# Setup of an attention and two-mixture kernel: outer rows set on chip, loads and constants in another order, narrower products of ones

## The chip, the cores and the metric

One Trainium2 chip, one of its cores. The metric is device time in microseconds (us) of one execution of the whole program.

## What is computed

Three parts follow one another; everything is float32. The change touches only what stands before the first one's loop.

```python
for t in range(S):                       # B=4, H=8, S=768, D=48
    kt, vt, rt = (k[:, :, t], v[:, :, t], r[:, :, t])
    cur = einsum('bhd,bhe->bhde', u * kt, vt)
    y[:, :, t] = einsum('bhd,bhde->bhe', rt, state + cur)
    state = w * state + einsum('bhd,bhe->bhde', kt, vt)
```

y becomes x (3072 tokens x 384). The first mixture forms softmax(x @ phi) over tokens and over slots, runs 32 slots through eight experts (384 to 1024 to 384) and mixes them back. The second sends each token to the expert of its largest x @ w_gate, scaled by that probability.

## The kernel before, in words

The recurrence is done in chunks of 128 tokens. Two heads with 48 features each sit on 96 of the 128 partitions (rows LO=16 to R2=112; the 16 rows on either side are unused), so there are 4 pairs of heads and 6 chunks, 24 steps (`pe_step`, L973), a loop of six chunks with four steps written out. In a step TensorE (PE) does `increments` (L932), `scores` (L920), the carried part (L943), `turn` (L963), `logits` (L968, with phi) and `within` (L954). Scores and within put their products on the four quadrants of the array in turn. Before a step VectorE (DVE) multiplies the loaded rows `ind` with a table of powers of w (`pre`, L637, giving `rkb`), and GpSimd (POOL) multiplies the token rows `intk` with the table's transpose `kttab` (L434, giving `kt`); ScalarE (ACT) multiplies by u (L486). `increments` waits for `kt` (L925), and POOL waits for `kttab`, `rkb` and the token rows (L429 to L432).

Setup has to bring this about, on five queues written out by hand; each engine runs its own in order.

- SyncE (SP), L309 to L323: w and u into `wusb` (96 rows, then the same small rows twice into the outer 16), the rows `ind` for steps 0 and 1 (`load_d`; step 0's misses the outer rows), four loads of phi, the gate's weights, token rows (`load_t`) and more `ind`.
- ACT, L462 to L467: waits for w and u, loads the outer rows of step 0's `ind` (`load_gaps`), loads its activation table, waits for the transposes and copies them to `kttab`.
- POOL, L412 to L423: the nine constants counted by `consts` (ones, ident, xs, two selects, fold, revi, sta, kt's margin), then `kt` of step 0.
- DVE, L606 to L650: memset of phi's unused rows, wait for all nine constants, masks, wait for w and u, six doublings of the table (L624 to L626, each on the last), `wk` (L642, L643), scaling of the table, `pre(0)`, `pre(1)`.
- PE, L888 to L901: 15 products of ones (`warm`, 128x128 each, their result unused), five products of xs that clear PSUM banks, the four transposes of `wk`, eight more products of ones, a wait for phi and the gate's weights, step 0.

Of the kernel before, what the change touches and what calls it, by code (L numbers as in the profile page):

```python
# [12 lines left out]
P = 128  # L13
# [6 lines left out]
R2 = HB + D  # L20
LO = HB - D
# [5 lines left out]
NS = E * SPE  # L27
# [8 lines left out]
def mixed_kernel(nc, dmaj, tmaj, wu, phi, wa, wg, wb, out):  # L36
    ctx = ExitStack()
    with ctx:
# [13 lines left out]
        def sem(name):  # L52
            return ctx.enter_context(nc.semaphore(name))
# [13 lines left out]
        xs = sb("xs", [P, B, C])  # L67
# [37 lines left out]
        ones = sb("ones", [P, P])  # L105
# [64 lines left out]

        zeroed = sem("zeroed")
        consts = sem("consts")
        wu_in = sem("wu_in")
        small_in = sem("small_in")
# [107 lines left out]
        PARTS = ((0, 3), (3, 6))  # L282
        NCONST = 9
# [7 lines left out]
        def _(sp):  # L291
            drows = dmaj.rearrange("n r i c -> (n r) i c")

            def load_d(n):

                row = (n // PAIRS + n % PAIRS * NC) * 2 * D  # L300
                if row >= LO and row + P - LO <= STEPS * 2 * D:
                    sp.dma_start(ind[:, n % 4, :, :], drows[row - LO:row - LO + P, 0:2]).then_inc(ind_in[n % 4], 16)
                else:
                    sp.dma_start(ind[LO:R2, n % 4, :, :], drows[row:row + 2 * D, 0:2]).then_inc(ind_in[n % 4], 16)

            def load_t(n):
                sp.dma_start(intk[:, n % 4, :, :, :], step_of(tmaj, n)).then_inc(tok_in[n % 4], 16)

            sp.dma_start(wusb[LO:R2, :, :], wu[:]).then_inc(wu_in, 16)  # L309
            sp.dma_start(wusb[0:LO, :, :], wu[0:LO]).then_inc(wu_in, 16)  # L310
            sp.dma_start(wusb[R2:P, :, :], wu[0:LO]).then_inc(wu_in, 16)
            load_d(0)
            load_d(1)
# [4 lines left out]
            sp.dma_start(wgsb[:, :, :], wg).then_inc(small_in, 16)  # L318
            load_t(0)
# [84 lines left out]
        def _(pool):  # L404
# [3 lines left out]
            def step(ins):  # L408
                n[0] += 1
                ins.then_inc(consts, 1)  # L410
# [3 lines left out]
            step(g.memset(xs[:, :, :], 0.0))  # L414
# [4 lines left out]
                                 base=0, pattern=[[-1, P]], channel_multiplier=1))  # L419
            step(g.memset(fold[:, :], 0.0))  # L420
# [28 lines left out]
        def _(sc):  # L449
# [12 lines left out]
            sc.wait_ge(wu_in, 48)  # L462
# [132 lines left out]
        def _(dve):  # L595
# [5 lines left out]
            def link(ins):  # L601
                chain[0] += 1
                ins.then_inc(dch, 1)
                dve.wait_ge(dch, chain[0])

            v.memset(phisb[32:64, :, :, :], 0.0).then_inc(zeroed, 1)  # L606
            v.memset(tab[:, :, 1, HALF - 1:HALF], 1.0)
            dve.wait_ge(consts, NCONST)
# [9 lines left out]
            dve.wait_ge(wu_in, 48)  # L618
# [10 lines left out]
            def scale_tables(a, b):  # L629
                inv = winv[0:P, a:b].unsqueeze(2).unsqueeze(3).to_broadcast([P, b - a, 2, HALF])  # L630
                return v.tensor_tensor(tab[0:P, a:b, :, :], tab[0:P, a:b, :, :], inv, ALU.mult)
# [13 lines left out]
            link(scale_tables(0, 1))  # L645
            pre(0)
# [231 lines left out]
        def _(pe):  # L878
# [4 lines left out]
            def warm(n, bank):  # L883

                for _ in range(n):
                    mm(ps[:, bank, 0:P], ones[:, :], ones[:, :], start=True, stop=True)  # L886

            pe.wait_ge(consts, 1)  # L888
            warm(15, SC)
            pe.wait_ge(consts, NCONST)  # L890

            for bank in (YB, YB + 1, SB, SB + 1, LB):
                mm(ps[:, bank, 0:B * HALF], xs[0:R2, 0, :], xs[0:R2, 0:2, :].rearrange("p b t -> p (b t)"),
                   start=True, stop=True)
            pe.wait_ge(wk_ready, 1)
# [4 lines left out]
            warm(8, SC)  # L900
            pe.wait_ge(small_in, 5 * 16)  # L901
# [210 lines left out]
            turn_c(4)  # L1112
            for k in range(KD):
                pe.wait_ge(sot_ready, k + 1)
                ins = mm(ps[:, 3, 0:E], sot[:, k, :], wgsb[:, k, :], start=(k == 0), stop=(k == KD - 1))
# [140 lines left out]
```

## Time and profile before

| | |
|---|---|
| median of three runs | 281.63 us (279.12 to 281.95) |
| profiled execution, its own time | 280.6 us |
| span of the profiled execution | 278.8 us |
| mean granted clock of TensorE | 0.978 of full speed |
| PE busy | 260.8 us, 94% of the span |
| DVE busy | 153.2 us, 55% |
| chain that ended last | PE 81%, DVE 13%, issue 3% |
| HBM read and written | 50.32 MB and 4.72 MB |

The span goes from the first to the last instruction. The granted clock is a share of 2.4 GHz. "issue" in a chain is time in which an engine waited for nothing that the profile shows. A product of ones or of xs is recorded as two instructions.

### The profile page before, as it was taken

To read this page: it belongs to the slowest core of one execution; us is meant where nothing else is said; L and a number is where in the kernel's file an instruction comes from. 1 tells how busy PE (TensorE), PEld (TensorE's weight loads), DVE (VectorE), ACT (ScalarE), POOL (GpSimd) and SP (SyncE) were. 2 spreads that over 40 slices of the span, in tenths; PEclk is the share of its full clock that TensorE was granted. 3 is DMA by queue.
4 is the path that set the end of the run, shared out by engine and by line. 5 is a ranking of instruction groups with operands and counts; after the bars stand their busy time and mean duration, and the time that the engine had idled before them with its cause. 6 is when DMAs were issued, how large, how long until landed. Compare 5 with 4: busy or idle time off the path is not lost.

```text
span 278.8 us, 10399 instructions
## 1 busy us (share of the span) xinstructions
PE 260.8 (94%) x4505; PEld 220.9 (79%) x4505; DVE 153.2 (55%) x296; ACT 88.7 (32%) x175; POOL 30.5 (11%) x45
## 2 busy tenths in 40 slices
PE   8989799989999998999999989999999999999992
PEld 8967687877788775433468679999999999999991
DVE  5787488888888876247021487342522524425203
ACT  1224254544555544030220273222222222222200
POOL 3222122222222124000000000000000000000000
PEclk9999799999999999999997799999999999999998
DMA  5975889999999999999804700030030300300303
GB/s 158 331 241 171 256 321 322 394 363 395 385 360 365 319 405 418 423 385 414 364 2 155 298 2 1 0 114 0 0 113 0 113 0 0 113 0 1 114 0 119
DMA packets 16324, 55.30 MB, mean 198 GB/s; under 512 B 1936, under 2 KB 5200, under 8 KB 15408
## 3 DMA queue, kind: packets, MB, share of 16 engines
q1 hardware_dynamic: 13216, 43.90, 42.6%
q10 hardware_dynamic: 3088, 11.14, 10.7%
q8 instruction: 12, 0.20, 0.3%
q14 instruction: 8, 0.07, 0.1%
HBM read 50.32 MB, written 4.72 MB: 197 GB/s over the span
## 4 chain that ended last, share of the span: by engine, by line
PE 81%; DVE 13%; issue 3%; ACT 1%; POOL 0%; DVEq 0%; POOLq 0%
PE ps L1183 12%; PE ps L1182 12%; PE ps L1184 12%; PE ps L920 9%; PE ps L954 6%; DVE pt L669 6%; PE ps L886 5%; DVE pt L666 5%; PE ps L932 4%; PE ps L1167 4%; PE ps L1054 4%; PE ps L1076 4%; PE ps L1023 2%; PE ps L1085 1%; PE ps L1124 1%
## 5 line engine op out<-in xcount | busy, mean ns | idle before, releaser
L1183 PE MATMUL ps<-w2l,hh 128*128 128x384 f32 x192 | 64.5, 336 | 0.0
L1182 PE MATMUL ps<-w2h,hh 128*128 128x384 f32 x192 | 64.4, 335 | 0.0
L821 DVE SCALAR_TENSOR_TENSOR hl<-ps,hh 128x512 fp32r<-128x512 f32 x48 | 32.9, 689 | 57.1 <-ACT hh L567 57.1
L1184 PE MATMUL ps<-w2h,hl 128*128 128x384 f32 x192 | 64.2, 335 | 0.0
L567 ACT ACTIVATE hh<-ps 128x512 fp32r<-128x512 f32 x48 | 28.7, 600 | 74.1 <-PE ps L1167 74.1
L1183 PEld LDWEIGHTS ps<-w2l,hh 128*128 128x128 f32 x192 | 36.0, 188 | 1.6
L1182 PEld LDWEIGHTS ps<-w2h,hh 128*128 128x128 f32 x192 | 36.0, 188 | 0.7
L1184 PEld LDWEIGHTS ps<-w2h,hl 128*128 128x128 f32 x192 | 36.1, 188 | 0.0
L434 POOL TENSOR_TENSOR kt<-intk,kttab 128x384 f32<-128x384 f32 x24 | 24.1, 1006 | 74.7 <-DVE rkb L637 50.0
L637 DVE TENSOR_TENSOR rkb<-ind,tab 128x1024 f32<-128x1024 f32 x24 | 29.9, 1246 | 1.4 <-DMA ind<-dmaj 1.3
L920 PE MATMUL ps<-rkb 64*64 64x128 f32 x768 | 27.5, 279 | 0.0
L666 DVE TENSOR_TENSOR pt<-ps,mask 128x512 f32<-128x512 f32 x24 | 16.6, 692 | 12.5 <-PE ps L920 12.5
L500 ACT ACTIVATE xs<-ps 112x512 f32<-112x512 f32 x24 | 14.3, 597 | 26.5 <-PE ps L954 26.5
L920 PEld LDWEIGHTS ps<-rkb 64*64 64x64 f32 x768 | 22.2, 135 | 0.0
L954 PEld LDWEIGHTS ps<-pt,intk 64*48 64x48 f32 x768 | 13.2, 119 | 11.3 <-issue 11.3
L943 PE MATMUL ps<-rkb,stb 64*48 64x64 f32 x384 | 21.0, 224 | 0.0
L954 PE MATMUL ps<-pt,intk 64*48 64x64 f32 x768 | 16.4, 220 | 4.7 <-DVE pt L669 3.6
L943 PE MATMUL ps<-rkb,sta 64*48 64x64 f32 x384 | 20.6, 224 | 0.0
L1167 PE MATMUL ps<-cs,gst 128*128 (+1 forms) x48 | 18.7, 395 | 1.6 <-DVE gst L809 1.1
L943 PEld LDWEIGHTS ps<-rkb,sta 64*48 64x48 f32 x384 | 15.6, 122 | 3.5 <-issue 0.3
L886 PE MATMUL ps<-ones 128*128 128x128 f32 x80 | 16.9, 372 | 1.3 <-POOL ident L413 1.3
L669 DVE COPY_PREDICATED pt<-diag,ps 128x512 f32<-128x512 int32 x24 | 17.6, 733 | 0.8
(163 smaller groups left out, 308.1 us busy)
## 6 DMA issues: line engine op xcount, KB each, us to landing
ind<-dmaj SPq DMA_DIRECT2D x22, 512.0 KB, 8.0
wearly<-wa ACTq DMA_DIRECT2D x21, 512.0 KB, 7.4
intk<-tmaj SPq DMA_DIRECT2D x24, 384.0 KB, 7.1
wearly<-wa SPq DMA_DIRECT2D x4, 1536.0 KB, 10.0
out<-acc SPq DMA_DIRECT2D x5, 768.0 KB, 3.6
wlate<-wa SPq DMA_DIRECT2D x4, 768.0 KB, 8.3
wlate<-wa SPq DMA_DIRECT2D x2, 1536.0 KB, 10.7
wmid<-wa SPq DMA_DIRECT2D x1, 1536.0 KB, 8.0
```

Of the source, the lines that this page charges most:

```text
L637: v.tensor_tensor(rkb[0:P, n % 4, 0:2, :].rearrange("p i (g t) -> p i g t", t=HALF), ind[0:P, n % 4, :, :].rearrange("p i (g t) -> p i g t ...
L666: v.tensor_tensor(pt[:, :, :, :], score[:, :, :, 0, :], causal, ALU.mult).then_inc(pt_ready, 1)
L669: v.copy_predicated(pt[:, :, :, :], on_diag, score[:, :, :, 1, :]).then_inc(att_ready, 1)
L821: v.scalar_tensor_tensor(out=hl[:, f % 4, :], in0=ps[:, f % 4, :], scalar=0.0, in1=hh[:, f % 4, :].bitcast(F32), op0=ALU.max, op1=ALU.subt ...
L886: mm(ps[:, bank, 0:P], ones[:, :], ones[:, :], start=True, stop=True)
L920: ins = mm(ps[toks[m], SC + j, b * C:(b + 1) * C], rkb[toks[j], ip, 1, at_], rkb[toks[j], ip, 0::2, at_], start=True, stop=True, skip_grou ...
L943: ins = mm(ps[rows[j ^ b % 2], YB + m, b * HALF:(b + 1) * HALF], st[toks[j], ip, b, :], rkb[toks[j], ip, 0, b * C + m * HALF:b * C + (m + ...
L954: ins = mm(ps[rows[j ^ b % 2], YB + m, b * HALF:(b + 1) * HALF], intk[toks[m], ip, 1, b, j * D:(j + 1) * D], pt[toks[m], j, b, :], start=F ...
L1167: mm(ps[:, f % 4, :], gst[:, f * P:(f + 1) * P], cs[:, bass.ds(u * (UT * P), UT * P)], start=True, stop=True).then_inc(h_done, 1)
L1182: mm(o, a_h, w2h[:, f, :], start=(f == 0), stop=False)
L1183: mm(o, a_h, w2l[:, f, :], start=False, stop=False)
L1184: ins = mm(o, a_l, w2h[:, f, :], start=False, stop=(f == KF - 1))
```

## The change

DVE sets the outer rows of `wusb` to 1.0 itself, in two memsets (rows 0 to 31 and 96 to 127), ahead of everything else, and signals it by `sides_set`; the two loads of these rows go. SP issues step 0's `ind` first, then waits for `sides_set`, then loads the 96 rows of w and u, then step 0's token rows; step 1's `ind` goes behind phi. The gate's weights get a semaphore of their own, for which PE waits only where it needs them. ACT no longer waits for w and u in front of the outer rows of `ind`. POOL sets xs behind the two selects, and DVE's masks wait for four constants instead of nine; the wait for nine stands in front of `pre(0)`. The products of ones shrink to 32x32, and 79 in three places stand where 23 stood in two.

```diff
+            load_d(0)
+            sp.wait_ge(sides_set, 1)
             sp.dma_start(wusb[LO:R2, :, :], wu[:]).then_inc(wu_in, 16)
-            sp.dma_start(wusb[0:LO, :, :], wu[0:LO]).then_inc(wu_in, 16)
-            sp.dma_start(wusb[R2:P, :, :], wu[0:LO]).then_inc(wu_in, 16)
-            load_d(0)
-            load_d(1)
+            load_t(0)
             sp.wait_ge(zeroed, 1)
...
-            sp.dma_start(wgsb[:, :, :], wg).then_inc(small_in, 16)
-            load_t(0)
+            load_d(1)
+            sp.dma_start(wgsb[:, :, :], wg).then_inc(wg_in, 16)
...
-            step(g.memset(xs[:, :, :], 0.0))
             pool.wait_ge(consts, n[0])
...
+            step(g.memset(xs[:, :, :], 0.0))
...
-            sc.wait_ge(wu_in, 48)
             load_gaps()
...
+            v.memset(wusb[0:32, :, :], 1.0)
+            v.memset(wusb[96:P, :, :], 1.0).then_inc(sides_set, 1)
             v.memset(phisb[32:64, :, :, :], 0.0).then_inc(zeroed, 1)
             v.memset(tab[:, :, 1, HALF - 1:HALF], 1.0)
-            dve.wait_ge(consts, NCONST)
+            dve.wait_ge(consts, NSHAPE)
...
-            dve.wait_ge(wu_in, 48)
+            dve.wait_ge(wu_in, 16)
...
             link(scale_tables(0, 1))
+            dve.wait_ge(consts, NCONST)
             pre(0)
...
-            def warm(n, bank):
+            def warm(n, bank, width=P):
 
                 for _ in range(n):
-                    mm(ps[:, bank, 0:P], ones[:, :], ones[:, :], start=True, stop=True)
+                    mm(ps[0:width, bank, 0:width], ones[:, 0:width], ones[:, 0:width], start=True, stop=True)
 
             pe.wait_ge(consts, 1)
-            warm(15, SC)
+            warm(24, SC, NS)
...
+            warm(28, SC, NS)
             pe.wait_ge(wk_ready, 1)
...
-            warm(8, SC)
-            pe.wait_ge(small_in, 5 * 16)
+            warm(27, SC, NS)
+            pe.wait_ge(small_in, 4 * 16)
...
             turn_c(4)
+            pe.wait_ge(wg_in, 16)
```

NSHAPE is 4, NS 32, P 128.

PE's instructions from the start up to step 0, first as they stood and then as they stand now. A row is a line of the kernel, the operation, what it writes and from what, its shape, and how many in a row; `ps<-ones` are the products of ones, `ps<-xs` those that clear banks, `ps<-ident,wk` the transposes.

```order
0 L877 UNCONDITIONAL_BRANCH
1 L886 MATMUL ps<-ones 128x128 x15
2 L893 MATMUL ps<-xs 128x256 x5
3 L897 MATMUL ps<-ident,wk 128x112 x4
4 L886 MATMUL ps<-ones 128x128 x8
5 L990 UNCONDITIONAL_BRANCH
```

```order
0 L881 UNCONDITIONAL_BRANCH
1 L890 MATMUL ps<-ones 32x32 x24
2 L897 MATMUL ps<-xs 128x256 x5
3 L890 MATMUL ps<-ones 32x32 x28
4 L902 MATMUL ps<-ident,wk 128x112 x4
5 L890 MATMUL ps<-ones 32x32 x27
6 L995 UNCONDITIONAL_BRANCH
```

A third group has come between the clearing products and the transposes, and all three are narrow.

SyncE's issues at the start, as they stood and as they stand now: `wusb<-wu` is w and u, `ind<-dmaj` the rows for DVE (96 or 128 partitions), `phisb<-phi` phi, `wgsb<-wg` the gate's weights, `intk<-tmaj` token rows.

```order
2 L309 DMA wusb<-wu 96x8
3 L310 DMA wusb<-wu 16x8
4 L311 DMA wusb<-wu 16x8
5 L304 DMA ind<-dmaj 96x1024
6 L302 DMA ind<-dmaj 128x1024
7 L316 DMA phisb<-phi 48x128 [waits zeroed]
8 L317 DMA phisb<-phi 48x128
9 L316 DMA phisb<-phi 48x128
10 L317 DMA phisb<-phi 48x128
11 L318 DMA wgsb<-wg 128x24
12 L307 DMA intk<-tmaj 128x768 x2
```

```order
2 L307 DMA ind<-dmaj 96x1024
3 L314 DMA wusb<-wu 96x8 [waits sides_set]
4 L310 DMA intk<-tmaj 128x768
5 L318 DMA phisb<-phi 48x128 [waits zeroed]
6 L319 DMA phisb<-phi 48x128
7 L318 DMA phisb<-phi 48x128
8 L319 DMA phisb<-phi 48x128
9 L305 DMA ind<-dmaj 128x1024
10 L321 DMA wgsb<-wg 128x24
11 L310 DMA intk<-tmaj 128x768
```

Step 0's rows have moved ahead of w and u, its token rows ahead of phi, and step 1's rows behind phi.

## Rows read from the trace of the kernel before

**Rows 1.** Chain of waits, first 40 us: start, us, what ran or was waited for.
```profile
1.27 6.36 PE ps L886 x30
7.63 2.16 PE ps L893 x10
9.79 0.38 PE ps L897 x4
10.17 1.80 PE ps L886 x16
...
12.09 0.62 PE ps L932 x23
...
19.82 0.75 issue
...
27.97 1.35 issue
```

**Rows 2.** Timeline, 0 to 24 us: start, us, engine, line, operation, out<-in, count, idle before.
```profile
3.21 0.87 ACTq L455 DMA_DIRECT2D ind<-dmaj  x2
3.21 0.17 DVE L613 TENSOR_TENSOR tab<-strict 128x4 f32<-128x4 f32 x1 [1.45 <-POOL kt L423]
...
4.04 0.16 DVE L619 TENSOR_TENSOR uw<-wusb 128x4 f32<-128x4 f32 x1
...
7.20 0.42 DVE L643 TENSOR_TENSOR wk<-tab,pw 128x256 f32<-128x256 f32 x1
...
7.47 2.32 PE L893 MATMUL ps<-xs 112*128 112x256 f32 x10
...
9.26 1.23 DVE L637 TENSOR_TENSOR rkb<-ind,tab 128x1024 f32<-128x1024 f32 x1 [1.32 <-DMA ind<-dmaj]
...
10.21 0.49 ACT L467 ACTIVATE kttab<-ps 128x384 f32<-128x384 f32 x1 [4.60 <-PE ps L897]
...
10.84 1.00 POOL L434 TENSOR_TENSOR kt<-intk,kttab 128x384 f32<-128x384 f32 x1 [7.66 <-ACT kttab L467]
...
15.31 0.66 PE L954 MATMUL ps<-pt,intk 64*48 64x64 f32 x32
...
15.77 0.76 PE L932 MATMUL ps<-intk,kt 64*64 64x48 f32 x32
```

**Rows 3.** Timeline of later steps, the same columns, 19 to 40 us.
```profile
24.01 0.99 PE L954 MATMUL ps<-pt,intk 64*48 64x64 f32 x32 [0.17 <-DVE pt L669]
...
30.38 0.62 PE L932 MATMUL ps<-intk,kt 64*64 64x48 f32 x30 [0.17 <-issue]
...
35.40 0.63 PE L932 MATMUL ps<-intk,kt 64*64 64x48 f32 x32
...
39.06 0.66 PE L932 MATMUL ps<-intk,kt 64*64 64x48 f32 x32
```

**Rows 4.** DMA view, 0 to 40 us: a queue's packets; issues by size, us to landing.
```profile
q8 instruction: 4, 0.07, 0.6%
...
ind<-dmaj SPq DMA_DIRECT2D x10, 512.0 KB, 5.7
...
ind<-dmaj SPq DMA_DIRECT2D x1, 384.0 KB, 4.2
...
phisb<-phi SPq DMA_DIRECT2D x4, 24.0 KB, 4.7
...
wusb<-wu SPq DMA_DIRECT2D x1, 3.0 KB, 1.6
```

**Rows 5.** Windows (PE, PEld, DVE, ACT, POOL busy, PEclk, DMA); line L1124.
```profile
31.00:32.00 1.00, 1.00 (x28) 1.00 (x24) 0.41 (x1) 0.49 (x1) 0.00 (x0) 0.50 0.94 156
147.00:150.40 3.40, 3.06 (x28) 3.06 (x28) 0.73 (x5) 0.29 (x1) 0.00 (x0) 1.00 0.07 18
150.50:153.00 2.50, 2.50 (x14) 2.50 (x13) 0.00 (x0) 0.00 (x0) 0.00 (x0) 0.50 0.90 344
...
L1124 PE MATMUL ps<-gw,cs x24: 252/253/354, 147.3 to 152.9; 128*128 128x8 f32 x24
```

More of the change, by code:

```diff
@@ L168, in mixed_kernel @@
         ltok = flat[:, 0:NC * P].rearrange("p (c b s) -> p c b s", c=NC, b=B)
+        sides_set = sem("sides_set")
         zeroed = sem("zeroed")
@@ L173, in mixed_kernel @@
         wu_in = sem("wu_in")
+        wg_in = sem("wg_in")
         small_in = sem("small_in")
@@ L282, in mixed_kernel @@
         PARTS = ((0, 3), (3, 6))
+        NSHAPE = 4
         NCONST = 9
```

## The prediction

> **What bounds the kernel now.** I read the chain of waits first, over the first 40 us [rows 1]: it is almost wholly TensorE (PE). PE runs products of ones from 1.27, five products of xs from 7.63, four transposes of the table from 9.79, eight more products of ones from 10.17, and begins step 0 at 12.09. The 15 products of ones are 30 records of an instruction, two per product, and last 6.36 us; the later eight, 16 records, last 1.80. One record costs 0.212 us in the first run and 0.112 in the second: PE began on its lower level, 1.2 GHz, and went over to 2.4 GHz. Solving 30 records over the 6.20 us from 1.27 to the first xs record at 7.47 [rows 2] for the two prices (28 slow, 2 fast) puts the change at 7.2 us; the granted clock, which reads 1.00 from the start, does not show it.
>
> The timeline of setup [rows 2] shows who else is near. VectorE (DVE) starts its table at 3.21, when GpSimd's (POOL) ninth constant is there, reaches the powers at 4.04, ends wk at 7.62, and then sits idle for 1.32 us until the first rows of ind land at 9.26; that product ends at 10.49. ScalarE copies the table from 10.21 to 10.70, POOL multiplies it into kt from 10.84 to 11.84, PE starts step 0 at 12.09. So two arms nearly tie for kt: PE's (transposes end 10.17, 1.92 us before step 0) and DVE's (product ends 10.49, 1.60 before). A shortened wait counts only if both move.
>
> After setup nothing in the change touches a step. A step undisturbed takes 3.66 us (35.40 to 39.06), and steps wait on PE and DVE by turns, not on setup [rows 3]. So what setup gains is carried to the end once. Span 278.8 plus 1.8 us around it make this execution's 280.6.
>
> **DVE's arm, part by part.** The wait for nine constants becomes a wait for four, and xs's memset goes behind the two selects, so the table's first product leaves 3.21 for about 2 us. Its masks are 0.83 us of work (3.21 to 4.04) and end before 3.2 even if that start were 2.4. What ends last is then w and u, whatever these edits bring. Before, their three loads went out first, landed 1.6 us after issue (the last at about 3.3) and cost nothing. Now the one load waits for two short memsets on DVE (issue about 1.55), and on SyncE's queue it stands behind 384 KB of ind issued at the program's start, 0.8. The queue gives small loads no way past: phisb's 24 KB loads, issued behind 896 KB of ind, took 4.7 us where wusb took 1.6 [rows 4]. The same 384 KB took 4.2 us. So w and u land at 0.8 + 4.2 = 5.0, plus an estimated 0.2 for the gap rows that ScalarE now issues at the same moment: 5.2. Were they held by nothing, 1.55 + 1.6 = 3.15; behind a load as slow as the whole ind rows (5.7), 6.5. I take 5.2, as its row is the same transfer.
>
> DVE so reaches the powers 1.16 us later than before (5.2 against 4.04). wk ends at 8.78, the table's first part is scaled by 9.1 (7.62 to 7.94 before, where the idle time begins). The wait for ind goes, as its three loads, issued at 0.8 to 1.2 instead of up to 3.65, are there by 6.9 even at 5.7 us each. The first product runs 9.12 to 10.35, and POOL can start 0.14 later (as 10.70 to 10.84): 10.49. Step 0 is 1.25 behind POOL's start: 11.74. What replaces the idle 1.32 is w and u: the DVE arm gains 0.2 to 0.35 and no more. The two ends of the landing would put step 0 at 9.7 and at 13.0.
>
> **PE's arm.** 15 products of 128 columns go, 24 of 32x32 come. No row shows such a product. Eight records follow one another in each quadrant of L954 (32 records on four): start to start of the next group 0.46 us, 0.0575 each for 64 columns, against half of 0.112 = 0.056 [rows 2]. So the price goes by columns, plus about 0.002: for 32 columns 0.030 a record, 0.06 a product at 2.4 GHz and 0.11 at 1.2. The other end is that narrowness saves nothing: L1124's moving side has 8 columns, yet the window it shares with 128-wide ones holds 28 records in 3.06 us, 0.109 each [rows 5]. Those have 128 columns to load, the new ones 32, so I stay by L954.
> - 24 x 0.11 = 2.64: PE reaches the xs products at 3.91 (the ninth constant comes at 3.2 as before, since POOL's total is unchanged).
> - They now run on the lower level, where they cost twice 2.16/5 = 0.43. Until 7.2 that is 3.29/0.86 = 3.8 products, then 1.2 x 0.43 = 0.50: end at 7.70 instead of 9.79.
> - 28 x 0.06 = 1.68: 9.38. wk is ready at 8.78, so these products are 0.6 too many here.
> - Transposes 0.38: 9.76, 0.41 us before the old 10.17. Copy, kt and step 0 follow 1.92 later: 11.68.
> - The last run is 27 x 0.06 = 1.62 instead of 1.80: it ends at 11.38, inside the wait for kt.
>
> The two arms give 11.74 and 11.68 against 12.09: **0.35 to 0.41 us gained**, 0.4 taken. If the small price is exact in columns (0.056), PE's arm is at 11.5 and DVE's decides; if the clock rises later, both kernels lose half of the delay.
>
> The Trainium skill, "TensorE: Matmul & The Clock Gate", section "The mechanism" of the part on packing small matmuls, says that a weight load overlaps running products only when the row group differs. All products of ones use the same rows. The trace disagrees: in 3.40 us of products of ones and of the gate, loads and products are each busy for 3.06 [rows 5]. By the rule, small loads and products would take turns; that is rival 2 below.
>
> **Other edits.** The moved load of ind for step 1 is issued at about 4.3 instead of 2.63, behind token rows and phi. Whole ind loads took 5.7 us, so it lands by 10.0; DVE wants it at 10.35 + 0.55 = 10.9. Cover is 0.9 us; gone, step 1 would wait that much. Token rows of step 0 are issued at about 2.0, ahead of phi: even at 5.7 they are there by 7.7, wanted at 10.5. SyncE issues two small loads fewer and waits once more, all off the path. phi is issued from 2.5 to 4.2, earlier than before by half a microsecond, and at 4.7 lands by 9, wanted at 11.4. The gate's own semaphore is passed 130 us after its load: 0. Rows of w set to one change no work. Unseen and not bounded by the order alone: 56 more products move the places at which PE's instruction queue is refilled. Three stalls that end for no releaser (0.75 at 19.82, some 0.3 in L954 at 24.01, where the group lasts 0.99 against 0.66, and 1.35 at 27.97) come while instruction packets are on the rings: four in 40 us [rows 3, 4]. After the last, the granted clock fell to 0.50 by 31 [rows 5], and step 4 lasted 5.02 (30.38 to 35.40), 1.36 over a free step. These bound what a shift could do: -0.75 - 1.35 - 1.36 = -3.5 to, with one stall and one slow step more, +2.7. I take 0, since a step has 72 products and the stalls stand a little under a step apart (19.82, within 24.01 to 25.00, 27.97), so 56 more in front moves each place by nearly one spacing, onto its neighbour's.
>
> The Trainium skill, "Runtime: NRT & Kernel Launch", section "Instruction fetch mechanics", says that an engine's instructions are refilled in blocks by transfers of their own, and that crossing a block's edge is mostly hidden. By that rule the shift costs nothing and the stalls are of another cause. No row settles it; 1.35 us is not hidden if it is a refill.
>
> **Rivals.**
> 1. The forecast: both arms by 0.4. 280.6 - 0.4 = 280.2; on the mean of the four executions shown (three times and the profiled one, 280.8) it is 280.4.
> 2. Small products take load and stream in turn: 0.12 a product, 0.22 slow. 24 x 0.22 to 6.55; xs to 9.0; 28 x 0.12 to 12.4; transposes to 12.8; 27 x 0.12 to 16.0, step 0 there instead of at 12.09: +3.9, 284.7. For it: no row shows narrow products one after another on the same rows. Against: L954. At no saving at all, 24 products end at 9.5, xs at 11.6, the rest at 24.2: +12, the end of that bound.
> 3. Slower by the clock: the small runs and the 0.3 us hole behind them fail to hold 2.4 GHz, the granted clock falls around step 0 and one step lasts 1.36 more. 280.8 - 0.4 + 1.36 = 281.8. It decides if PE is off 2.4 GHz at 12 us. For it: in 147 to 150.4 PE was busy for 3.06 of 3.40 us, every second product or so with 8 columns moving, and the clock was at 0.50 from 150.5 all the same [rows 5]. Against: the first run of ones raised it, and load and product are equally wide in both kinds.
> 4. Refills fall elsewhere: all three losses gone, 280.4 - 3.5 = 276.9; or one stall and slow step more, 283.1.
> 5. w and u are not held by ind: DVE's arm is at 9.7, but PE's stays at 11.68, so again 280.4. That the change does less than meant on DVE hides behind PE, and the other way round.
>
> **How the numbers follow.** Forecast (with rival 5) 0.53; rival 2 0.06; rival 3 0.18; rival 4 faster 0.15, slower 0.08. Time 280.4. The likeliest's own range is 279.2 to 281.6, the scatter of its arms and of the executions. The range leaves out rival 2 and the outer edge of rival 4: 277.6 to 283.0. A measurement of this kernel can tell about 1% from no change: faster by over 1% is rival 4's good side and a little of the forecast's scatter, 0.18; slower by over 1%, rival 2 and part of rival 4, 0.11; within, 0.71.
>
> **What would show it.** Right: DVE's uw starts at 5.0 to 5.5 with ind's load of 96 rows just landed; no idle before the first rkb; xs products from 3.9 with long records; about 0.06 us a small product after 7.2; step 0's L932 group at 11.6 to 11.8; then steps of 3.66. Wrong: uw before 4.5 and step 0 before 11.3; transposes later than 10.2; a granted clock of 0.50 before 20 us; stalls without a releaser that sum to 1 us more or less than 2.4.

## The result, and the profile after

The change made the kernel slower: 283.62 us median of 20 executions (281.68 to 287.15) against 281.29 of 20 before (277.12 to 282.35). The ratio is 1.0119, 95% interval 1.0092 to 1.0146. A ratio is made of the undisturbed executions alone, a median of all, so the two can point apart. The profiled execution took 283.61, its span 281.9, its mean granted clock 0.979: 3.0 above the one of before, so it stands for the medians' 2.3 with 0.7 of scatter.

Lines have moved: products of ones are L890 (before L886), xs L897, transposes L902, increments L937 (L932), scores L925, the carried part L948, logits L973, within L959 (L954), `kt` L436, `rkb` L640. The timeline of the changed kernel's setup, columns as in [rows 2]:

```profile
1.27 2.74 PE L890 MATMUL ps<-ones 128*32 128x32 f32 x48 [1.27 <-POOL ident L415]
...
3.94 4.00 PE L897 MATMUL ps<-xs 112*128 112x256 f32 x10
...
5.22 0.16 DVE L622 TENSOR_TENSOR uw<-wusb 128x4 f32<-128x4 f32 x1 [2.03 <-DMA wusb<-wu]
...
7.87 1.96 PE L890 MATMUL ps<-ones 128*32 128x32 f32 x56
...
9.16 1.22 DVE L640 TENSOR_TENSOR rkb<-ind,tab 128x1024 f32<-128x1024 f32 x1
9.75 0.60 PE L902 MATMUL ps<-ident,wk 112*128 112x112 f32 x4
...
10.89 1.23 DVE L640 TENSOR_TENSOR rkb<-ind,tab 128x1024 f32<-128x1024 f32 x1
11.02 2.90 POOL L436 TENSOR_TENSOR kt<-intk,kttab 128x384 f32<-128x384 f32 x2 [7.76 <-ACT kttab L468]
```

Up to here it is nearly the forecast's setup. The wait of DVE for the first rows of `ind` is gone, and a wait of 2.03 us for w and u stands in its place. What the forecast does not have is the last row's length: two `kt` products one behind the other, 2.90 us. The line's own view gives their durations, shortest, median and longest in ns, and who waited:

```profile
L436 POOL TENSOR_TENSOR kt<-intk,kttab x2: 994/1468/1943, 11.0 to 12.9; 128x384 f32<-128x384 f32 x2
...
  PE ps L937: 1.0, 1
```

The chain of waits of the changed kernel, 0 to 45 us (columns as in [rows 1]), says where the rest is:

```profile
9.82 0.55 PE ps L902 x4
...
11.02 1.95 POOL kt L436
...
13.22 0.62 PE ps L937 x23
...
17.43 0.45 PE ps L937 x23
17.88 2.17 issue
20.05 0.20 PE ps L937
...
28.02 0.66 PE ps L959 x31
28.68 0.53 issue
29.21 0.25 PE ps L959
...
32.66 0.44 PE ps L959 x14
33.11 0.62 issue
```

Step 0 starts at 13.22 instead of 12.09. Then PE stops three times for nothing that the profile shows, once for 2.17 us behind the 31st of the 32 records of `increments` of step 1; before it was 0.75, 0.3 and 1.35 at other places [rows 1, 3]. The windows of those microseconds, columns as in [rows 5]:

```profile
17.00:18.00 1.00, 0.88 (x62) 0.75 (x53) 1.00 (x1) 0.49 (x1) 0.00 (x0) 1.00 1.09 385
18.00:19.00 1.00, 0.00 (x0) 0.00 (x0) 0.05 (x1) 0.81 (x2) 0.87 (x1) 1.00 0.78 311
...
20.00:21.00 1.00, 0.91 (x24) 0.74 (x27) 0.41 (x1) 0.00 (x0) 0.00 (x0) 0.90 0.02 8
21.00:22.00 1.00, 1.00 (x32) 1.00 (x26) 0.11 (x1) 0.00 (x0) 0.00 (x0) 0.50 0.08 16
```

The stall begins while `ind` and token rows fill the DMA engines (385 and 311 GB/s), and behind it the granted clock falls to 0.50. So step 1 lasts from 17.22 to 24.79, 7.57 us: a free step of 3.66, the stall of 2.17 and 1.74 more. Step 5, where the rows of `increments` show both kernels running freely again (after, then before at 35.40 in [rows 3]):

```profile
38.18 0.66 PE L937 MATMUL ps<-intk,kt 64*64 64x48 f32 x32
```

That is 2.78 us later than before: 1.13 of it stood at step 0, 1.65 came in steps 0 to 4. The 1.65 is a difference of two rounds that both have stalls: the stalls sum to 3.3 against 2.4, the step with the clock at 0.50 costs 1.74 against 1.36, and step 0 lasts 4.00 against 3.68. Nearly the whole 3.0 of the two profiled executions is therefore there by 38 us.

### The profile page after: what moved, and what is told of

Read it like the earlier page. It is cut to its first block, busy times and chain, and to the rows that moved or that the text cites. A ratio compares the mean times of both kernels' runs of the same rounds, so it can differ in the third digit from the quotient of the medians.

```text
span 281.9 us, 10624 instructions
## 1 busy us (share of the span) xinstructions
PE 260.9 (93%) x4617; PEld 219.4 (78%) x4617; DVE 153.6 (54%) x298; ACT 88.8 (32%) x175; POOL 31.4 (11%) x45
## 4 chain that ended last, share of the span: by engine, by line
PE 76%; DVE 14%; issue 4%; DMA 2%; ACT 1%; POOL 1%; SPq 1%; DVEq 0%; POOLq 0%
PE ps L1189 12%; PE ps L1188 12%; PE ps L1190 12%; PE ps L925 9%; DVE pt L673 6%; PE ps L959 6%; DVE pt L670 6%; PE ps L937 4%; PE ps L1173 4%; PE ps L1059 4%; PE ps L1081 4%; DMA wraw<-wb 2%; PE ps L890 2%; PE ps L1028 2%; PE ps L897 1%
## 5 line engine op out<-in xcount | busy, mean ns | idle before, releaser
L1189 PE MATMUL ps<-w2l,hh 128*128 128x384 f32 x192 | 65.2, 340 | 0.0
L1188 PE MATMUL ps<-w2h,hh 128*128 128x384 f32 x192 | 65.1, 339 | 0.0
L1189 PEld LDWEIGHTS ps<-w2l,hh 128*128 128x128 f32 x192 | 36.6, 191 | 1.7
L1188 PEld LDWEIGHTS ps<-w2h,hh 128*128 128x128 f32 x192 | 36.6, 191 | 0.7
L436 POOL TENSOR_TENSOR kt<-intk,kttab 128x384 f32<-128x384 f32 x24 | 25.0, 1043 | 76.4 <-DVE rkb L640 53.2
L640 DVE TENSOR_TENSOR rkb<-ind,tab 128x1024 f32<-128x1024 f32 x24 | 29.2, 1219 | 0.1
L925 PE MATMUL ps<-rkb 64*64 64x128 f32 x768 | 27.7, 277 | 0.1
L925 PEld LDWEIGHTS ps<-rkb 64*64 64x64 f32 x768 | 22.1, 134 | 2.8 <-issue 2.8
L959 PEld LDWEIGHTS ps<-pt,intk 64*48 64x48 f32 x768 | 13.3, 119 | 11.4 <-issue 11.4
L959 PE MATMUL ps<-pt,intk 64*48 64x64 f32 x768 | 16.5, 220 | 5.2 <-DVE pt L673 4.1
L948 PE MATMUL ps<-rkb,stb 64*48 64x64 f32 x384 | 21.1, 225 | 0.0
L948 PE MATMUL ps<-rkb,sta 64*48 64x64 f32 x384 | 20.8, 225 | 0.0
L1173 PE MATMUL ps<-cs,gst 128*128 (+1 forms) x48 | 19.6, 416 | 1.1 <-DVE gst L813 0.7
L937 PE MATMUL ps<-intk,kt 64*64 64x48 f32 (+1 forms) x768 | 16.0, 212 | 4.4 <-issue 3.3
L948 PEld LDWEIGHTS ps<-rkb,sta 64*48 64x48 f32 x384 | 15.7, 122 | 3.5 <-issue 0.3
```

What stands on the lines that cost most here:

```text
L640: v.tensor_tensor(rkb[0:P, n % 4, 0:2, :].rearrange("p i (g t) -> p i g t", t=HALF), ind[0:P, n % 4, :, :].rearrange("p i (g t) -> p i g t ...
L925: ins = mm(ps[toks[m], SC + j, b * C:(b + 1) * C], rkb[toks[j], ip, 1, at_], rkb[toks[j], ip, 0::2, at_], start=True, stop=True, skip_grou ...
L948: ins = mm(ps[rows[j ^ b % 2], YB + m, b * HALF:(b + 1) * HALF], st[toks[j], ip, b, :], rkb[toks[j], ip, 0, b * C + m * HALF:b * C + (m + ...
L959: ins = mm(ps[rows[j ^ b % 2], YB + m, b * HALF:(b + 1) * HALF], intk[toks[m], ip, 1, b, j * D:(j + 1) * D], pt[toks[m], j, b, :], start=F ...
L1173: mm(ps[:, f % 4, :], gst[:, f * P:(f + 1) * P], cs[:, bass.ds(u * (UT * P), UT * P)], start=True, stop=True).then_inc(h_done, 1)
L1188: mm(o, a_h, w2h[:, f, :], start=(f == 0), stop=False)
```

## The experiments

Two things are to be told apart: the hold of `kt` on POOL, and the stalls without a releaser. My theory of the stalls was that they are refills of PE's instruction queue, at fixed counts of products; its rival, that they come from the moment, by what the loads and the other engines do then. "In front" below is the number of products of any kind before step 0: 32 before the change (15 + 5 + 4 + 8) and 88 after (24 + 5 + 28 + 4 + 27). A step has 72: 16 of `increments`, 16 of `scores`, 8 carried, 4 of `turn`, 8 carried, 4 of `logits`, 16 of `within`, each recorded twice but for the four of `turn`. Each ratio is to the kernel before, run beside the kernel in question.

**e1_hold**: DVE's second product is kept behind POOL's first.

```diff
+            dve.wait_ge(kt_ready, 1)
             pre(1)
```

> The changed kernel, with DVE made to wait for kt of step 0 before its second ind product. Theory A (the first kt product took 1.94 us instead of 1.00 because DVE's second ind product, started 0.13 us ahead of it, kept it from working): the first kt product lasts 1.00 again and step 0 starts at about 12.25 instead of 13.22; the second ind product ends at about 13.3 instead of 12.1. The time falls by about 1.0 us against the changed kernel. Rival R (that product was long for another reason, late token rows or its first use): it stays at 1.9 us, and step 0 starts at 13.2 or later. Either way the stall of about 2.2 us in increments of step 1 stays.

Measured: 283.09 us, ratio to before 1.0144 (1.0077 to 1.0211). Its timeline of setup:

```profile
10.42 0.49 ACT L468 ACTIVATE kttab<-ps 128x384 f32<-128x384 f32 x1 [7.21 <-PE ps L903]
...
11.05 1.00 POOL L436 TENSOR_TENSOR kt<-intk,kttab 128x384 f32<-128x384 f32 x1 [7.79 <-ACT kttab L468]
12.14 1.23 DVE L640 TENSOR_TENSOR rkb<-ind,tab 128x1024 f32<-128x1024 f32 x1 [1.18 <-issue]
```

`kt` takes 1.00 again, and step 0 comes at 12.30, 0.92 earlier. Before the change the same pair met the other way round, and it was DVE's product that became long (timeline of the kernel before, behind POOL's start at 10.84 in [rows 2]):

```profile
10.98 1.93 DVE L637 TENSOR_TENSOR rkb<-ind,tab 128x1024 f32<-128x1024 f32 x1
```

So whichever of the two starts first is done in its own time (1.23 or 1.00), and the other ends 0.85 (POOL behind DVE) or 1.07 us (DVE behind POOL) after it. 0.13 us of order decides over 0.94 us of `kt`. Yet the kernel is no faster: its chain has stalls of 2.18 at 13.43 and 1.90 at 19.12.

**e2_refill** and **e3_both**: eight products more in the third run, without and with e1's wait.

```diff
-            warm(27, SC, NS)
+            warm(35, SC, NS)
```

> The changed kernel with 35 instead of 27 small products in the third run, so 64 instead of 56 more products than before in front of step 0. Theory B (PE's instructions are refilled every 64 products, and where the boundary falls in a step sets the stall): the stalls return to the places of the kernel before: about 0.75 at the end of within of step 1, some 0.3 in within of step 2, about 1.35 in logits of step 3, and the 2.17 in increments of step 1 is gone. Step 0 still starts near 13.2 (the third run ends about 12.8). Steps 1 to 4 last together about 1 to 1.5 us less than in the changed kernel. Rival R (stalls come from the DMA traffic of these moments, not from the place in the program): the 2.2 us stall stays in increments of step 1, and the time is the same or worse by the eight products.

> Both edits of e1 and e2 together. Theories A and B: step 0 at about 12.8 to 13.0 (the third run of ones now ends about 12.8 and decides), stalls at the old places; the time is about 1.5 to 2 us under the changed kernel and equal to the kernel before within 1 us. If neither theory holds: as the changed kernel.

Measured: 282.91, ratio 1.0133 (1.0071 to 1.0195), and 283.68, ratio 1.0116 (1.0044 to 1.0188). The stalls moved and the 2.17 is gone: e2 stands still for 1.68 in front of `scores` of step 0 (its chain counts 1.02 of it, at 13.65), 1.29 at 22.29 and 0.76 at 32.05. That sums to 3.7 against 3.3, so nothing was saved. With 96 in front the edges, the products at which a refill is due, lie at the old places within the steps, but each is a later piece of the program than before. A miss for "the places alone decide".

**e4_wu_first**: w and u issued ahead of step 0's `ind`.

```diff
-            load_d(0)
             sp.wait_ge(sides_set, 1)
             sp.dma_start(wusb[LO:R2, :, :], wu[:]).then_inc(wu_in, 16)
+            load_d(0)
```

> The changed kernel with w and u loaded ahead of step 0's ind instead of behind it. Theory C (w and u were held by the 384 KB in front of them, and the DVE arm follows their landing): uw starts at about 3.2 instead of 5.22, wk ends at 6.8, the first ind product at about 8.5. PE's arm stays (transposes at 9.75, kt product from 11.0), and as DVE's second ind product is over before or soon after 11.0, kt needs 1.0 to 1.4 us: step 0 at 12.3 to 12.7 instead of 13.22. Rival R (w and u land late for another reason, such as the wait for the memsets): uw stays near 5.

Measured: 283.49, ratio 1.0186 (1.0124 to 1.0248). The powers start at 3.53 instead of 5.22, so the 384 KB in front did hold this load; `wk` is there by 7.1, step 0 starts at 11.90. Then `increments` of step 1 stalls for 2.18 again, and nothing of the 1.3 us is left in the median.

**e5_pe_alone** and **e6_rest_alone** split the change: the kernel before with the new products of ones only, and the change without them (15 and 8 wide ones as before). **e12_rest_again** is e6 again, on another chip.

> The kernel before with only PE's products changed (24, 28 and 27 narrow ones in three places). Theory B, now as e1 to e3 left it (an instruction refill is asked for when PE passes an edge, every 64 products, and is there 4 to 6 us later; 79 quick products in setup use one up early, so the first round of the loop is paced by refills whatever the other arms do): step 0 starts at about 12, stalls stand in scores of step 0 or increments of step 1 as in the changed kernel, step 5 starts near 38 instead of 35.4, and the time is 2 to 3 us over before, nearly all of the change's loss. Rival A (the loss is DVE's second ind product holding up kt, which needs the DVE side of the change): here kt comes first as before, so the time is that of before.

> The change without PE's part: 15 and 8 products of 128 columns as before, all the rest changed. Theory B: stalls where the kernel before has them (end of within of step 1, within of step 2, logits of step 3), step 5 within 0.7 us of 35.4, time within 1 us of before; uw at about 5.2. Step 0 at 12.1 if kt starts ahead of DVE's second ind product, at 13.1 if behind it, and then 0 to 1 us longer in all. Rival: the moved loads cost the time; then this kernel is as slow as the changed one, and step 0 or a later step waits on DMA.

> The same kernel as e6 (the change without PE's part), for a profile without a disturbed clock and to bound its gain, as it measured 1.1% under before. Expected: 0.5 to 1.3% under before again. If the gain is from setup, step 0 starts before 12.0; if it is from the stalls, steps 1 to 4 together last under 22 us against 23.3 before.

Measured: e5 283.47, ratio 1.0108 (1.0045 to 1.0171); e6 279.43, ratio 0.9891 (0.9843 to 0.9939); e12 280.64, ratio 1.0019 (0.9915 to 1.0122). The new products of ones, by themselves, lose as much as the whole change. The rest gives nothing that holds up: e6's 1% did not come back. The chain of e5, in which setup's loads are those of before:

```profile
12.61 0.51 PE ps L921 x15
13.12 0.59 issue
...
16.77 0.45 PE ps L933 x23
17.22 2.18 issue
19.40 0.20 PE ps L933
...
28.05 0.97 issue
```

The same product of step 1 stalls for the same 2.18, at another time (17.22) and behind other loads. That is the sign of a count, not of a moment.

**e7_few_wide**: seven long products instead of the 79, which keep PE busy with less of its program (16 in front; `width` columns read from one column of ones).

```diff
-                    mm(ps[0:width, bank, 0:width], ones[:, 0:width], ones[:, 0:width], start=True, stop=True)
+                    mm(ps[:, bank, 0:width], ones[:, :], ones[:, 0:1].to_broadcast([P, width]), start=True, stop=True)
...
-            warm(24, SC, NS)
+            warm(3, SC, 256)
...
-            warm(28, SC, NS)
+            warm(2, SC, 512)
...
-            warm(27, SC, NS)
+            warm(2, SC, 512)
```

> The changed kernel with its 79 narrow products replaced by 7 wide ones of about the same length (3 of 256 columns, then 2 and 2 of 512), so 16 products stand in front of step 0 instead of 88. Theory B: the first edge falls at the end of scores of step 0 and only three refills stand in the loop's first round instead of five; stalls of about 1 us each near step 1's scores, step 2's and step 3's, step 5 at 35 to 36, time 2 to 3.5 us under the changed kernel, at or under before. Rival A: step 0 is again held by kt (13.1) and the time stays that of the changed kernel.

Measured: 286.41, ratio 1.0173 (1.0109 to 1.0237), the slowest of the timed kernels: "fewer products, fewer stalls" fell. Timeline of e7 (PE), and its windows:

```profile
16.60 0.66 PE L925 MATMUL ps<-rkb 64*64 64x128 f32 x14
19.04 0.70 PE L925 MATMUL ps<-rkb 64*64 64x128 f32 x17 [1.78 <-issue]
...
21.95 0.66 PE L937 MATMUL ps<-intk,kt 64*64 64x48 f32 x30
26.39 0.32 PE L937 MATMUL ps<-intk,kt 64*48 64x48 f32 x2 [3.78 <-issue]
```

```profile
23.00:24.00 1.00, 0.00 (x0) 0.00 (x0) 0.00 (x0) 0.53 (x1) 0.85 (x1) 1.00 0.80 320
24.00:25.00 1.00, 0.00 (x0) 0.00 (x0) 0.00 (x0) 0.00 (x0) 0.00 (x0) 1.00 0.00 0
25.00:26.00 1.00, 0.00 (x0) 0.00 (x0) 0.00 (x0) 0.00 (x0) 0.00 (x0) 0.71 0.00 0
26.00:27.00 1.00, 0.61 (x10) 0.56 (x13) 0.26 (x1) 0.00 (x0) 0.00 (x0) 0.50 0.00 0
```

From 24 to 26 every engine and every DMA engine is idle. One instruction packet (the DMA view's q8) starts between 23.80 and 23.95, when the loads are through, and PE goes on 2.4 to 2.6 us later. The clock falls within that idle time.

**e8_no_middle**: no second run (60 in front).

> The changed kernel without the 28 products of the middle run, so 60 in front of step 0. Transposes follow wk at about 8.9 instead of 9.75, kt starts near 10.5 ahead of DVE's second ind product, step 0 at about 11.8. Theory B: the first edge is passed in the third run (about 10.3), so step 0 stalls near its turn (about 15.3) and step 5 starts near 36, some 2 us less than the changed kernel. Rival A alone: no stall but those of before, 1.4 us less than the changed kernel. Rival C (the middle run is needed to hold the clock): the granted clock reads 0.50 somewhere from 9 to 16 us and step 0 is longer by over 1 us.

Measured: 282.87, ratio 1.0057 (1.0017 to 1.0098), step 0 at 12.95. Its windows show what the second run is good for:

```profile
8.00:9.00 1.00, 0.00 (x0) 0.00 (x0) 0.93 (x5) 0.00 (x0) 0.00 (x0) 1.00 1.25 356
9.00:10.00 1.00, 0.81 (x4) 0.60 (x4) 0.93 (x3) 0.00 (x0) 0.00 (x0) 0.65 0.74 284
10.00:11.00 1.00, 1.00 (x19) 0.94 (x19) 1.00 (x2) 0.74 (x2) 0.04 (x1) 0.50 0.99 368
```

PE is idle for 1.87 us before the transposes, from 7.32; the clock goes down in the slice from 9 to 10 and stays at 0.50 into 12 us.

**e9_mixed** (24 narrow, then 4 and 8 products of 128 columns; 45 in front) and **e10_mixed_wu_first** (the same with e4's order of loads):

```diff
-            warm(28, SC, NS)
+            warm(4, SC)
...
-            warm(27, SC, NS)
+            warm(8, SC)
```

> The changed kernel with its first run left at 24 narrow products, its middle run of 28 narrow ones made 4 of 128 columns and its third of 27 made 8 of 128 columns: the same lengths in time (0.89 and 1.8 us), but 45 products in front of step 0 instead of 88. Theory B (what costs is the number of products, since PE's instructions come in pieces of 64 products and each piece needs 2.3 us and its wait on the rings): edges fall at places 3 and 67 of step 0, then late in steps 1 to 3, four pieces in the first round instead of five; stalls sum to 2 to 2.7 us, none over 1.5; step 5 at 34.5 to 36; the time is 2 to 4 us under the changed kernel and equal to or under before. Rival R (narrow products cost by something else than their number, for instance the clock they hold): the first run is still narrow, so the time stays within 1 us of the changed kernel.

> e9 with w and u also loaded ahead of step 0's ind. DVE's arm: uw at 3.5, first ind product from about 7.5, second from about 9.5 when its rows land. PE's arm: transposes at about 8.2 to 9, kt from about 9.5, 1.0 us if it starts ahead of DVE's second ind product and up to 1.4 if behind. Step 0 at 10.6 to 11.5, about 1 us before e9's. Theory B with refills paced by the ring: part of that microsecond is given back in stalls; the time is 0 to 1 us under e9. If stalls did not follow, the full microsecond shows.

Measured: 280.3, ratio 1.0029 (0.9966 to 1.0092), and 280.76, ratio 1.0053 (0.9989 to 1.0116). Step 0 starts at 12.14 and 10.28: 1.86 us of a shorter setup bring nothing. Step 5 starts at 36.02 and 34.72.

**e11_long_run**: 91 narrow products in the third run, so that the count passes an edge where PE waits for no data. This is the most direct of the runs.

```diff
-            warm(27, SC, NS)
+            warm(91, SC, NS)
```

> The changed kernel with 91 instead of 27 narrow products in its third run, 64 more, to see a refill by itself. Theory B: the second edge lies after the 51st product of that run, where no step and no other engine plays a part; PE stops there for 1 to 2.5 us in the middle of like instructions, until some 2.3 us after an instruction packet starts on the rings. The next edge is at the 24th product of step 0 with one more stall of 1 to 2 us. Rival R (the stalls come from what the steps wait for): the run of 91 goes through in 6.4 us without a gap.

One execution, 287.86. Timeline of e11, and of its DMA view the window 11.9 to 12.0 (a queue's packets, MB, share of the engines):

```profile
9.95 3.48 PE L890 MATMUL ps<-ones 128*32 128x32 f32 x104
14.37 2.65 PE L890 MATMUL ps<-ones 128*32 128x32 f32 x78 [0.94 <-issue]
...
20.80 0.66 PE L937 MATMUL ps<-intk,kt 64*64 64x48 f32 x31
24.17 0.24 PE L937 MATMUL ps<-intk,kt 64*48 64x48 f32 x1 [2.72 <-issue]
```

```profile
q8 instruction: 1, 0.02, 58.4%
```

Between two like products with nothing between them PE stands still for 0.94 us, behind the 52nd of the run (104 records of two a product), which is the 113th of the program (24 + 5 + 28 + 4 + 52). The packet starts 2.4 us before PE goes on. The products there wait for no data and no other engine, and the granted clock reads 1.00 from 12 to 15. Counted the same way from records, give or take one where records are missing, every long stall lies 64 products, or a multiple of 64, from the others:

| kernel | in front | stall at | products up to it |
|---|---|---|---|
| after | 88 | 17.88 | 88 + 72 + 15.5 = 175.5 |
| after | 88 | 28.68 | 88 + 144 + 71.5 = 303.5 |
| after | 88 | 33.11 | 88 + 216 + 56 + 7 = 367 |
| e5 | 88 | 13.12 | 88 + 16 + 7.5 = 111.5 |
| e7 | 16 | 17.26, 22.61 | 16 + 72 + 16 + 7 = 111, 16 + 144 + 15 = 175 |
| e11 | 152 | 13.43, 21.45 | 113, 152 + 72 + 15.5 = 239.5 |

About 112, 176, 240, 304, 368: the same edges in every kernel, and the number in front says which product of a step they hit. The Trainium skill, "Runtime: NRT & Kernel Launch", section "Instruction fetch mechanics", gives a block as 16 KiB or 256 instructions. At two loads and two products for a float32 product that is the 64 seen here, and the packets have 0.02 MB: on the size the runs agree. The section also says that crossing an edge is mostly hidden; here it was not, with 0.94 us inside a run and 3.78 in a step.

**e13_old_places** (32 in front as before, made of 3 x 256, 2 x 512 and 1 x 512 columns and 17 narrow ones) and **e14_old_places_wu_first** (the same with e4's order):

```diff
-            warm(24, SC, NS)
+            long(3, SC, 256)
...
-            warm(28, SC, NS)
+            long(2, SC, 512)
...
-            warm(27, SC, NS)
+            long(1, SC, 512)
+            warm(17, SC, NS)
```

> The changed kernel with its runs of ones kept at about their lengths in time but made of 3 products of 256 columns, 2 of 512, and 1 of 512 with 17 narrow ones: 32 products in front of step 0, as before, instead of 88. Theory B' (the loss is where the refill edges fall in the steps: 64 products apart, and an edge at place 16 of a step after step 0 costs about 2 us or more, since it is asked for right behind the wait for DVE and while the next step's rows are on the rings): edges at 8, 72, 64 and 56 as before; no stall of over 1.6 us; time within 1% of before, 2 to 4 us under the changed kernel. Rival (the small and quick run itself costs, or the loads' new order): the time stays by the changed kernel's.

> e13 with w and u loaded ahead of step 0's ind. Step 0 at 10.3 to 10.8 against 12.1 in the kernel before. Theory B': edges as before, so 0.5 to 1.5 us under before, the rest given back where a refill comes later than the step. If it is the same as e13, all that setup gains is given back to the refills.

Measured: 281.08, ratio 1.0006 (0.9975 to 1.0037), and 279.18, ratio 0.9974 (0.9939 to 1.001). The chain of e14:

```profile
11.54 0.62 PE ps L943 x24
...
23.16 0.89 issue
...
27.51 0.53 issue
```

The old number in front gives the old time, with the new loads and the new order of constants. (e2 and e3 have the old places too, and not the old time.) The two stalls of e14 are 1.42 in all, step 5 starts at 32.79, and its median is the lowest of all, 1.8 below that of before as run beside it. By the ratio the gain is not proved: its interval includes 1.

**e15_before_moved**: the kernel before with 24 in front (11 of 128 and 2 of 256 columns, then 2 of 512 in place of 8), nothing else.

> The kernel before with nothing changed but how its ones are cut: 11 of 128 columns and 2 of 256 instead of 15 of 128, and 2 of 512 instead of 8 of 128; the same time, but 24 products in front of step 0 instead of 32, so every edge comes eight places later: 24 of step 0, 16 of step 1, 8 of step 2, 0 and 64 of step 3. Theory B': a stall of about 2 us or more in increments of step 1 as in the changed kernel, step 0 unchanged at 12.1, and 1 to 3 us over before. Rival (what costs is the number of products in front): fewer of them, so the same time as before or less.

Measured: 282.41 against 280.97 by the medians, but the ratio is 0.9964 (0.9922 to 1.0005). Half of the forecast failed. With 24 in front the edges lie at the same places of a step as with 88, yet nothing stands still at place 16 of step 1, where the changed kernel loses 2.17; a stall of 3.58 comes at 20.14, one edge later (24 + 144 + 7 = 175), in `increments` of step 2. So stalls keep to the edges, but the place in a step does not set the price of one, and by the ratio this kernel is not slower than before.

The timed kernels side by side. "Step 0" and "step 5" are the starts of their `increments`, "lost" is what five steps took over five free ones, 18.3, and "packets" are those of PE's queue in the whole execution; these four are read from the one profiled execution, whose time stands beside them and can lie well off the median (e2, e14):

| kernel | in front | packets | step 0 | step 5 | lost | profiled | median | ratio |
|---|---|---|---|---|---|---|---|---|
| before | 32 | 12 | 12.09 | 35.40 | 5.0 | 280.6 | 281.3 | 1 |
| e13 | 32 | 12 | 12.70 | 33.95 | 3.0 | 281.9 | 281.1 | 1.0006 |
| e14 | 32 | 12 | 11.54 | 32.79 | 3.0 | 276.4 | 279.2 | 0.9974 |
| e6 | 32 | 12 | 12.36 | 34.72 | 4.1 | 281.9 | 279.4 | 0.9891 |
| e12 | 32 | 12 | 12.10 | 34.35 | 4.0 | 279.2 | 280.6 | 1.0019 |
| e9 | 45 | 12 | 12.14 | 36.02 | 5.6 | 282.1 | 280.3 | 1.0029 |
| e10 | 45 | 12 | 10.28 | 34.72 | 6.1 | 281.7 | 280.8 | 1.0053 |
| e8 | 60 | 13 | 12.95 | 36.37 | 5.1 | 282.0 | 282.9 | 1.0057 |
| after | 88 | 13 | 13.22 | 38.18 | 6.7 | 283.6 | 283.6 | 1.0119 |
| e1 | 88 | 13 | 12.30 | 38.99 | 8.4 | 284.0 | 283.1 | 1.0144 |
| e4 | 88 | 13 | 11.90 | 36.91 | 6.7 | 283.0 | 283.5 | 1.0186 |
| e5 | 88 | 13 | 11.99 | 37.71 | 7.4 | 283.0 | 283.5 | 1.0108 |
| e2 | 96 | 13 | 12.31 | 37.56 | 7.0 | 286.5 | 282.9 | 1.0133 |
| e3 | 96 | 13 | 12.40 | 39.18 | 8.5 | 284.2 | 283.7 | 1.0116 |
| e15 | 24 | 12 | 12.26 | 37.55 | 7.0 | 284.3 | 282.4 | 0.9964 |
| e7 | 16 | 12 | 12.45 | 40.08 | 9.3 | 285.4 | 286.4 | 1.0173 |

Four kernels with 88 in front start step 0 at anything from 11.90 to 13.22 and have medians of 283.1 to 283.6. The number in front groups the ratios: within 0.6% of before from 24 to 60 (apart from e6's 0.9891, which did not come back), 1.1% to 1.9% over it at 88 and 96. The start of step 0 does not. e7, with 16, fits no such order. What comes behind the loop plays no part in this: it took 169.5 to 173.0 us in all sixteen, 171.1 before and 171.6 after.

The packets say more on why the number counts. PE's queue over the whole execution (packets, MB, share of the engines), first before, then after:

```profile
q8 instruction: 12, 0.20, 0.3%
```

```profile
q8 instruction: 13, 0.21, 0.3%
```

In the first 45 us, the first round of the loop and a little more, they start at 13.5, 18.1, 22.2 and 27.0 before, and at 11.9, 17.7, 21.9, 26.8 and 31.3 after; the next ones come at 65.0 and 67.3. The ones at about 18, 22 and 27 serve the same three edges in both, at nearly the same times, and PE gets past the edge near product 304 at 29.32 before and at 29.21 after. But after, 56 of these products were ones in place of work of the steps. At 3.66 us for the 72 products of a free step, 56 are 2.85 us (an estimate); step 5 came 2.78 later. My reading is that in this round the packets set the pace as well as the engines, and that a shorter setup (e1, e4) is given back there. No run shows it by itself, and the estimate is a rough one: it is right to 0.5 us for e8 and e9 and off by over a microsecond for e2, e4 and e10, the four other kernels with 32 in front reach step 5 by 0.7 to 2.6 before the kernel before does, and for e15 and e7 it has the wrong sign.

## Why the prediction was wrong

I forecast 280.4, no change; it was 283.6, slower by 1.2%. Two steps failed.

1. **"I take 0, since a step has 72 products and the stalls stand a little under a step apart"**: the term for the shifted refills. The observation was right and what I made of it wrong. The spacing is 64 products; 56 more in front is one spacing less 8, so the places are the neighbours' to within 8 products. But that like places cost alike is what failed: e2 and e3 have exactly the old places, one spacing on, and are 1.2% to 1.3% slower, and e15 has the places of the changed kernel and is not. What the shift did was to put 56 products of ones into the pieces that the first round is fed with. In the changed kernel that showed as 2.17 us at the end of `increments` of step 1 and, behind it, a clock of 0.50. The term measured +1.65 over steps 0 to 4 in the profiled execution, within the bound of +2.7 that I gave and then set aside. e5, which has the products of ones and not the hold of `kt`, is 1.1% slower by itself, and e13, which has the rest of the change and the old number, is not slower (1.0006).
2. **"POOL can start 0.14 later ... Step 0 is 1.25 behind POOL's start"**: this took `kt` at its 1.00. It lasted 1.95, since DVE's second `ind` product had started 0.13 us before it. That is 0.95 of step 0's delay against the forecast of 11.74. The other 0.53 is PE's arm. It was to end its transposes at 9.76 and ended them at 10.37: xs 0.2 longer, 28 narrow products at 0.07 instead of 0.06, the transposes at 0.55 instead of 0.38. The near tie of the two arms, which I described, was the reason to ask what the engines do to each other there. I asked only which is last. But step 0's delay was not what the time went by: e1 and e4 took 0.9 and 1.3 of it back and stayed at 283. So this is a second wrong step and not the one that lost the time.

Of the rest:

- "What setup gains is carried to the end once" failed with step 1: e10 starts step 0 by 1.86 us sooner than e9, and its ratio is 1.0053 against 1.0029.
- w and u held behind 384 KB: forecast 5.2, measured 5.22; e4's 3.53 shows that it is the order on the queue. Rival 5 is out. That the number came out so well is in part luck: the 384 KB took 3.2 us and not 4.2, and w and u landed 1.2 behind them and not 0.2.
- `wk` at 8.78: measured 8.80. First `ind` product 9.12: 9.16. The wait for `ind` gone: so it was.
- xs from 3.91 on the lower level: 3.94, 4.00 us long. 24 products at 0.11: 2.74 us, 0.114 each.
- Rival 2 is out: 28 narrow products take 1.96 us, with loads busy for 1.85 of them. The rule of the Trainium skill weighed there ("TensorE: Matmul & The Clock Gate", "The mechanism"), that a weight load overlaps running products only when the row group differs, does not hold for these products, which all use the same rows.
- Rival 3, the clock around step 0: it read 1.00 until 20. In the changed kernel it fell behind the stall of 2.17, not behind the narrow products.
- Rival 4's slower side, "one stall and slow step more", 283.1, is nearest to what happened: refills falling elsewhere, and 0.5 us off its time. I gave it 0.08. The faster side needed the stalls to vanish; the smallest sum in these runs is the 1.42 us of e13 and e14.
- The other edits (token rows ahead of phi, step 1's `ind` behind it, the gate's semaphore): 0 is within what the runs tell, by ratios of 0.9891 (e6) and 1.0019 (e12) for one and the same kernel.
- Signs named ahead: a clock of 0.50 before 20 us did not come (20.8); stalls more than 1 us off 2.4 did not come by their sum, 2.17 + 0.53 + 0.62 = 3.3, and yet the loss was there: a sign that counts only the stalls misses the 56 products that the packets carry besides the work.

What stays open: what sets the price of one refill. e7, with the fewest products, was the slowest, and e15, with 24, has the second longest stall and no loss by its ratio. The longest stalls are those whose packet starts only about when PE is at the edge or later: 17.7 for 17.88 (after), 21.24 for 20.14 (e15), 23.89 for 22.61 (e7). When a packet is asked for is not in the traces: e15's of 13.54 starts some 56 products ahead of its edge. That packets queue behind `ind` and token rows fits e7's and e15's windows, but no run varied the loads in those microseconds, so it is argued and not shown.

## What to carry to other kernels

Filler instructions on PE are not free even where they are hidden: 56 more of them cost 1.1% by themselves (e5), by my reading because the refills of its instruction queue then bring that much less work. Where steps follow that share the DMA queues with large loads, keep the number of products in front of them when only the filler's length is to change (e13: longer products, not more). Fewer is no rule either (e7: 1.7% slower with 16). Where POOL and DVE both read two operands from SBUF at the same time, decide their order rather than leave it to 0.1 us. And a shorter setup is worth only what the refills behind it leave: 1.86 us of it brought nothing in e10.

## What the runs showed of the hardware

- A refill's cost: a packet starts 2.3 to 2.5 us before PE goes on (after: 17.7 against 20.05; e11: 11.93 against 14.37; e7: 23.89 against 26.39). Over all stalls of 0.3 us or more in the first 43 us of the 17 kernels it is 2.2 to 2.9, with one of 3.6 (e7, at 35.97). A refill in a run of like products of 0.067 us leaves 0.94 uncovered.
- The loop's instructions come in its first round: before, PE's queue has a packet at 27.0, then one at 65.0 and none until 121, while the loop lasts to 107.7; after, at 31.3, 67.3 and 125, and the loop lasts to 110.3.
- POOL and DVE take turns for whole instructions: 1.00 becomes 1.94 behind DVE's 1.23, and 1.23 becomes 1.93 behind POOL's 1.00. The Trainium skill has it, "SBUF — State Buffer", section "Who interferes with whom": a DVE instruction with two SBUF inputs contends with a POOL instruction that reads SBUF, the shared port pair is an exclusive lock, and the order of issue decides who blocks. The trace agrees, and I had not applied it.
- The granted clock fell to 0.50 during or behind idle stretches of PE of 1.35 (before, at 31), 1.87 (e8), 2.17 (after) and 3.78 us (e7), and stayed at 1.00 through and behind one of 1.78 (e7, to 22).
